# Score products of the later batches: from one fp32 product per step to one stacked fp32r product per head

## The chip, the cores and the metric

The kernel runs on one core of one Trainium2 chip. The metric is the device time of one execution in microseconds (us), as the median of several runs. The core has TensorE (PE; its weight loads are shown apart as PEld), VectorE (DVE), ScalarE (ACT), GpSimd (POOL) and SyncE (SP), whose queue issues nearly all DMAs here.

## The reference

Per batch (4) and head (8) a gated linear attention with a running state over 768 tokens of 40 features, then a mixer over tokens and one over channels. Cut to what is computed:

```python
for t in range(S):
    m_new = max(f[t] + m, i[t]);  f_stab = exp(f[t] + m - m_new);  i_stab = exp(i[t] - m_new)
    C = f_stab * C + i_stab * outer(v[t], k[t]);  n = f_stab * n + i_stab * k[t]
    y[t] = sigmoid(o[t]) * (C @ q[t]) / max(|n . q[t]|, 1)
x = y as [batch, 768, 320]
u = x + (relu(x^T @ w_tok1) @ w_tok2)^T          # 768 -> 256 -> 768
out = u + relu(u @ w_ch1) @ w_ch2                # 320 -> 1536 -> 320
```

## The kernel before

**Attention in steps.** The recurrence is computed in chunks of L = 128 tokens (NC = 6 chunks), and within a chunk in NG = 3 groups of heads (3, 3 and 2 heads). One group of one chunk is a step; a batch has STEPS = 18 of them, numbered m. In batches 1 to 3 (the second to the fourth; the code counts from 0) a step m of batch `ba` goes as follows:

- PE `step_scores`: keys x queries of the group into one PSUM bank. Keys lie in `kd` (heads stacked over partitions, 120 rows); the queries lie in `qz`, zeros outside each head's own rows, so that one fp32 product of 384 (256) columns gives all heads of the step.
- DVE `scores` multiplies the bank by the decay weights in `gb` (which POOL `mask` and ACT `exps` made) and gives p_ready.
- The result is split into three bf16 pieces: ACT `p_high` (first piece), POOL `rest` (subtract it, then cast the second piece), DVE `p_low` (third piece, L860), semaphore p_split.
- PE `step_state` (L1075) adds to the state; DVE `state` fades and adds it.
- PE `step_values` works on step m - 2: the inter-chunk product (L1099) and six bf16 products per head (L1120), after p_split of that step.

Once per chunk come: ACT `chunk_start` (exp of the query decays `gq`, first piece of the values) and `v_middle`, POOL `weigh` (L517), the rest of the values (L551, L556), `scale_q` (queries times decays, L507), `mask` (L499, three) and `x_low` (L521), and DVE `values` (five small instructions).

**Where the steps lie.** Attention of the first batch is a stage of its own (to about 50 us of the span). The mixer of batch b then runs with the attention of batch b + 1 woven in by hand, in the same places on every engine. The channel mixer has 24 slots; in slot s PE does `hidden(s)` (8 fp32r products of 384 columns, L1222 to L1227), then attention step m = s + 2 of the next batch (s - 3 during the first batch's mixer), then `project(s - 1)` (9 fp32r products of 320 columns, L1151). ACT (`h_hi`, L755) and DVE (`h_lo`, L974) split the hidden values in each slot; each engine does its slot's split before its part of the attention step, in strict order. For b > 0, steps 0 and 1 lie in the token mixer before the slots. Steps 0 to 17 and the two values steps after them end in slot 17 (slot 22 of the first batch's mixer); the slots behind have only the mixer. During the first half of the first batch's slots ACT and DVE also split weights (L588, L841).

**Matrix products.** Mixer products are sums of three fp32r products of high and low halves. fp32r halves come from an ACT copy (high) and a subtract (low).

**POOL's order** for a chunk c, written out in `attention` of the POOL block: `weigh(c)`, values' rest, `rest(3c)`, `scale_q(c)`, values' third piece, `rest(3c+1)`, `mask(c+1)`, `rest(3c+2)`, `x_low(c-1)`.

**Loads.** SP issues everything in one order, each load behind the wait for its buffer. `load_chunk(ba, c)` is `load_scores` (keys and three parts of `qz`, 360 KB, buffers of 2 chunks), decays `gb` (3 buffers), `kv` (2), query decays `gq` (3) and queries `qd` (2).

Of the kernel before, what the change touches and what calls it, by code (L numbers as in the profile page):

```python
# [30 lines left out]
GH = 3  # L31
# [20 lines left out]
Q = 3  # L52
SEGMENTS = [(0, 1), (1, 3), (3, NC)]
# [28 lines left out]
def program(nc, qT, kT, kvN, i_gate, f_gate, o_gate, w_tok1, w_tok2, w_ch1, w_ch2, out):  # L82
    ctx = ExitStack()
    with ctx:
# [23 lines left out]

        qd = sb("qd", [ROWS, R, NG, L])
        kd = sb("kd", [ROWS, R, NG, L])  # L110
        qz = sb("qz", [ROWS, R, NG, GH, L])
        kv = sb("kv", [128, R, KV])
        vw = sb("vw", [128, 2, H, E1])

        with ExitStack() as early:
            carry_all = early.enter_context(nc.sbuf_tensor("carry", [NH, S], F32))
        vb = sb("vb", [128, 2, 3, H, E1], BF16)
        gb = sb("gb", [128, Q, H, L])
        gq = sb("gq", [ROWS, Q, NG, L])
        pb = sb("pb", [128, NG, 3, GH, L], BF16)  # L120
# [7 lines left out]
        gp = sb("gp", [3 * NH, S], BF16)  # L128
        g_mid = sb("g_mid", [NH, S], BF16)
        eye = sb("eye", [128, 128], BF16)  # L130
        above = sb("above", [128, L], BF16)
        pick = sb("pick", [3 * NH, NH], BF16)
        pick_q = sb("pick_q", [3 * NH, NG * GH, D], BF16)
# [12 lines left out]
        rows_p = pb[0:NH, :, :, :, :].rearrange("p r a h t -> p (r a h t)").bitcast(F32)  # L146
        f_row, i_row = rows[:, 0:S], rows[:, S:2 * S]
        G_row, A_row = rows_p[:, 0:S], rows_p[:, S:2 * S]
# [15 lines left out]

        def scores_bank(ba, m):

            return [pS, pC[0]][m % 2] if ba == 0 else pS
# [12 lines left out]
        gq_in = [sem(f"gq_in{i}") for i in range(Q)]  # L180
# [109 lines left out]
        def gq_fills(ba, c):  # L290

            return (ba - 1) * (1 if c % Q == 0 else 2) + (1 if c <= Q else 2)
# [11 lines left out]
        def _(sp):  # L304
# [3 lines left out]
            def load_scores(ba, c):  # L308

                n = NC * ba + c  # L310
                r = c % R
                if n >= R:
                    sp.wait_ge(s_mm, NG * (n - R + 1))
                ready = qk_in[r]
                queries = qT[ba, c]
                sp.dma_start(kd[:, r], kT[ba, c]).then_inc(ready, 16)
# [26 lines left out]
            def load_inter(ba, c):  # L343
# [3 lines left out]
                if ba > 0:  # L347
                    last_ba, last_c = (ba, c - Q) if c > Q else (ba - 1, c if c == Q else c + Q)
# [942 lines left out]
```

## Time and profile before

| | us |
|---|---|
| median of 3 runs | 457.97 (457.73 to 460.65) |
| profiled execution: time | 460.83 |
| profiled execution: span | 459.1 |
| TensorE's granted clock, mean | 0.996 of full |

The span is from the first to the last instruction in the trace; the time of that execution is 1.7 us more. The profile gives for each engine the busy time, a chain of work that ended last (followed back from the last instruction to what released each step), groups of instructions by line, and for each group the idle time before it. TensorE is clocked at its full level (2.4 GHz) in every stretch used here.

### The profile page before, as it was taken

The numbers are of one execution on the slowest core, as the hardware profiler recorded it, in microseconds if no ns is written. First come the engines' busy times: TensorE is split into PE (matmuls) and PEld (weight loads), VectorE is DVE, ScalarE is ACT, GpSimd is POOL, SyncE is SP. The second block draws the span as 40 slices with busy tenths as digits, with TensorE's granted clock in tenths as the row PEclk, the third lists the DMA queues.
The fourth block names the chain that finished last, engine by engine and source line by source line (L and its number), as shares of the span: only waits on it lengthen the run. The fifth ranks groups of instructions, "written<-read, shape, count | busy, mean of one in ns | idle before, by whom it ended". The sixth has DMA issues, their size and how long they took to land.

```text
span 459.1 us, 9511 instructions
## 1 busy us (share of the span) xinstructions
PE 440.7 (96%) x3463; PEld 407.9 (89%) x3463; DVE 259.1 (56%) x592; ACT 209.4 (46%) x517; POOL 209.1 (46%) x293
## 2 busy tenths in 40 slices
PE   7899989998999998999999998999999998999996
PEld 3587878998999997999999997899999997999996
DVE  8588965678865346776663236677674326222212
ACT  3665449665555247655552136755552213211120
POOL 7524410888886242988871204698883000000000
PEclk9899999999999999999999999999999999999999
DMA  7666991343344414544344013444410010000101
GB/s 215 191 172 192 348 256 39 104 115 129 95 134 136 140 44 115 148 127 131 127 152 141 1 44 87 144 135 140 126 60 1 1 43 1 0 2 0 45 1 43
DMA packets 36617, 47.38 MB, mean 103 GB/s; under 512 B 3357, under 2 KB 29083, under 8 KB 36571
## 3 DMA queue, kind: packets, MB, share of 16 engines
q1 hardware_dynamic: 35674, 45.76, 33.1%
q10 hardware_dynamic: 896, 1.02, 0.6%
q8 instruction: 28, 0.46, 0.4%
q14 instruction: 19, 0.15, 0.1%
HBM read 42.73 MB, written 4.03 MB: 102 GB/s over the span
## 4 chain that ended last, share of the span: by engine, by line
PE 83%; issue 6%; DVE 4%; ACT 3%; POOL 2%; DMA 1%; ACTq 0%; DVEq 0%; POOLq 0%
PE pC L1151 32%; PE pA L1222 7%; PE pA L1223 7%; PE pA L1224 7%; PE pS L1063 6%; PE pA L1151 5%; PE pY L1120 4%; PE pA L1226 3%; PE pA L1227 3%; PE pY L1099 2%; PE pN L1075 2%; DMA x<-o_gate_dram 1%; PE pA L1181 1%; POOL vw L517 1%; DVE pb L860 1%
## 5 line engine op out<-in xcount | busy, mean ns | idle before, releaser
L974 DVE SCALAR_TENSOR_TENSOR h_lo<-pA,h_hi 128x384 fp32r<-128x384 f32 x96 | 53.5, 557 | 148.0 <-ACT h_hi L755 147.9
L755 ACT ACTIVATE h_hi<-pA 128x384 fp32r<-128x384 f32 x96 | 46.9, 489 | 138.7 <-PE pA L1227 138.6
L1151 PE MATMUL pC<-wc_hi,h_hi 128*128 128x320 f32 x288 | 94.1, 327 | 0.8 <-DVE wc_lo L841 0.8
L1151 PE MATMUL pC<-wc_lo,h_hi 128*128 128x320 f32 x288 | 88.7, 308 | 0.0
L1151 PE MATMUL pC<-wc_hi,h_lo 128*128 128x320 f32 x288 | 88.5, 307 | 0.0
L489 POOL TENSOR_TENSOR gb<-gb,pb 128x384 f32<-128x384 f32 (+1 forms) x54 | 51.7, 957 | 65.7 <-ACT pb L623 65.4
L1222 PE MATMUL pA<-uT_hi,wc_hi 128*128 128x384 f32 x192 | 65.3, 340 | 1.9 <-DVE uT_hi L952 1.9
L1223 PE MATMUL pA<-uT_lo,wc_hi 128*128 128x384 f32 x192 | 64.7, 337 | 0.0
L1224 PE MATMUL pA<-uT_hi,wc_lo 128*128 128x384 f32 x192 | 64.3, 335 | 0.0
L1151 PEld LDWEIGHTS pC<-wc_hi,h_hi 128*128 128x128 f32 x288 | 54.0, 188 | 2.1 <-DVE h_lo L974 1.1
L1151 PEld LDWEIGHTS pC<-wc_lo,h_hi 128*128 128x128 f32 x288 | 54.2, 188 | 0.1
L1151 PEld LDWEIGHTS pC<-wc_hi,h_lo 128*128 128x128 f32 x288 | 54.0, 188 | 0.0
L613 ACT ACTIVATE gb<-gb,aT 128x128 f32<-128x128 f32 x144 | 47.6, 392 | 1.5 <-POOL gb L499 1.5
L1063 PE MATMUL pS<-qz,kd 120*128 120x384 f32 (+1 forms) x126 | 47.1, 454 | 0.0
L623 ACT ACTIVATE pb<-gb 128x384 bf16<-128x384 f32 (+1 forms) x54 | 26.4, 489 | 36.0 <-DVE gb L851 35.5
L860 DVE TENSOR_TENSOR pb<-gb,pb 128x384 bf16<-128x384 f32 (+1 forms) x54 | 38.6, 716 | 0.1
L1222 PEld LDWEIGHTS pA<-uT_hi,wc_hi 128*128 128x128 f32 x192 | 36.0, 187 | 3.0 <-DVE uT_hi L952 2.9
L521 POOL TENSOR_TENSOR x_lo<-x,x_hi 128x320 fp32r<-128x320 f32 x24 | 21.5, 896 | 33.4 <-ACT x_hi L647 33.4
L1224 PEld LDWEIGHTS pA<-uT_hi,wc_lo 128*128 128x128 f32 x192 | 36.0, 188 | 0.0
L1223 PEld LDWEIGHTS pA<-uT_lo,wc_hi 128*128 128x128 f32 x192 | 36.0, 188 | 0.0
L499 POOL TENSOR_SCALAR_AFFINE_SELECT gb<-gb 128x384 f32<-128x384 f32 (+1 forms) x54 | 29.8, 581 | 5.9 <-DMA gb<-g_dram 5.9
L851 DVE TENSOR_TENSOR gb<-pS,gb 128x384 f32<-128x384 f32 (+1 forms) x63 | 31.8, 504 | 1.1 <-PE pS L1063 0.8
(128 smaller groups left out, 885.0 us busy)
## 6 DMA issues: line engine op xcount, KB each, us to landing
gb<-g_dram SPq DMA_DIRECT2D x18, 512.0 KB, 4.0
kv<-kvN_dram SPq DMA_DIRECT2D x24, 324.0 KB, 4.1
kd<-kT_dram SPq DMA_DIRECT2D x24, 180.0 KB
qz<-qT_dram SPq DMA_DIRECT2D x72, 60.0 KB
out_dram<-u SPq DMA_DIRECT2D x24, 160.0 KB, 1.9
qd<-qT_dram SPq DMA_DIRECT2D x20, 180.0 KB, 2.6
gq<-g_dram SPq DMA_DIRECT2D x45, 60.0 KB
wc_raw<-w_ch_dram SPq DMA_DIRECT2D x6, 384.0 KB, 5.8
```

The source lines that it names most:

```text
L489: nc.gpsimd.tensor_tensor(tile, tile, pb[:, g, 0, 0:HEADS[g], :], ALU.subtract).then_inc(p_rest, 1)
L499: nc.gpsimd.affine_select(out=tile, in_=tile, compare_op=ALU.is_ge, fill=NEG, base=0, pattern=[[0, HEADS[g]], [1, L]], channel_multiplier= ...
L613: last = nc.scalar.activation(tile, tile, ACT.Exp, bias=aT[:, c, bass.ds(head, 1)])
L755: nc.scalar.activation(h2[0][:, slot % 2], pA[slot % 2][:, 0:HALF], ACT.Relu).then_inc(h2_hi, 1)
L851: nc.vector.tensor_tensor(tile, scores_bank(ba, m)[:, 0:n * L].rearrange("p (h t) -> p h t", h=n), tile, ALU.mult).then_inc(p_ready, 1)
L860: nc.vector.tensor_tensor(pb[:, g, 2, 0:n, :], gb[:, c % Q, GH * g:GH * g + n, :], pb[:, g, 1, 0:n, :], ALU.subtract).then_inc(p_split, 1)
L974: nc.vector.scalar_tensor_tensor(h2[1][:, slot % 2], pA[slot % 2][:, 0:HALF], 0.0, h2[0][:, slot % 2].bitcast(F32), ALU.max, ALU.subtract) ...
L1063: mm(scores_bank(ba, m)[:, 0:n * L], kd[0:n * D, r, g, :], qz[0:n * D, r, g, 0:n, :].rearrange("p h t -> p (h t)"), start=True, stop=True) ...
L1151: ins = mm(dst, a[p], b[q], start=first and n == 0, stop=last and n == 2)
L1222: mm(dst, wc1[0][:, t, f], uh[:, t, cols], start=t == 0, stop=False)
L1223: mm(dst, wc1[0][:, t, f], ul[:, t, cols], start=False, stop=False)
L1224: mm(dst, wc1[1][:, t, f], uh[:, t, cols], start=False, stop=False)
```

## The change

Batch 0 stays as it was (`first_scores`). For batches 1 to 3:

- **Data.** A new input `kq` holds, per batch, chunk and group, keys and queries head by head, 120 rows each. By features the stack is 0:40, 0:24, 0:40, 24:40, for keys and queries alike. Once rows 0 to 39 of the keys and rows 64 to 103 of the queries are replaced by their low halves, one product over the 120 rows sums low x high, high x low and (rows 40 to 63 and 104 to 119) high x high of a head.
- **Per step.** SP loads 120 x 768 floats (360 KB) into `kq_raw` (one buffer per group, so three). ACT `step_high` copies them to `kq_stack` as fp32r. POOL `low_keys` subtracts in rows 0 to 39, DVE `step_low` in rows 64 to 103. PE `step_scores` waits for both and then makes one fp32r product of 128 columns per head.
- **Where.** Step k is prepared two steps ahead (`prepares`): at m = 2 step 3, at m = 3 steps 4 and 5, then step m + 2; at m = 16 to 18 steps 0 to 2 of the next batch. The first three steps of batch 1 are prepared by POOL alone (`prepare_first`).
- **Loads.** `load_chunk` is now decays, two steps, values, third step, query decays, queries. `gq` has two buffers instead of three from batch 1 on; the first batch has `gq_first` as its third. Of batch 1 only chunk 0 is loaded ahead of `load_o(1)`, not two chunks.
- **Memory.** `qz`, `kd` and tensors that only the first batch uses lie under the new ones.

```diff
+FIRST_PREPARED = 3
+PREPARES_AT = 2
+TWO_AT = 3
+K_LOW, Q_LOW = slice(0, D), slice(64, 64 + D)
...
+        kq_raw = sb("kq_raw", [ROWS, NG, 2, GH, L])
+        kq_stack = sb("kq_stack", [ROWS, NG, 2, GH, L], F32R)
...
+        def prepares(ba, m):
+
+            if m < PREPARES_AT:
+                return []
+            steps = [m + 1] if m < TWO_AT else [m + 1, m + 2] if m == TWO_AT else [m + 2]
+            n = STEPS + (FIRST_PREPARED if ba < B - 1 else 0)
+            return [later(ba, k) for k in steps if k < n and later(ba, k) >= FIRST_PREPARED]
...
+            def load_step(ba, m):
+
+                c, g = divmod(m, NG)
+                k = later(ba, m)
+                if k < NG:
+                    sp.wait_ge(s_mm, STEPS)
+                elif k < NG + FIRST_PREPARED:
+                    sp.wait_ge(kq_first, 2 * (k - NG + 1))
+                else:
+                    sp.wait_ge(kq_lo, k - NG - FIRST_PREPARED + 1)
+                    sp.wait_ge(kq_low_keys, k - NG - FIRST_PREPARED + 1)
+                sp.dma_start(kq_raw[:, g], kq[ba - 1, c, :, g]).then_inc(kq_in[g], 16)
...
+            def load_two_steps(ba, c):
+                load_decays(ba, c)
+                load_step(ba, NG * c)
+                load_step(ba, NG * c + 1)
+
             def load_rest(ba, c):
-                if ba > 0:
-                    load_decays(ba, c)
                 load_values(ba, c)
+                load_step(ba, NG * c + 2)
                 if c > 0:
-                    load_inter(ba, c)
+                    load_query_decays(ba, c)
+                    load_queries(ba, c)
...
             def rest(ba, m):
 
+                sixteen_bits(ba, m)
+                for k in prepares(ba, m):
+                    low_keys(k)
...
+            def low_keys(k):
+
+                raw, stack = step_tiles(kq_raw, k % NG), step_tiles(kq_stack, k % NG)
+                pool.wait_ge(kq_hi, k - FIRST_PREPARED + 1)
+                nc.gpsimd.tensor_tensor(stack[0][K_LOW], raw[0][K_LOW], stack[0][K_LOW].bitcast(F32),
+                                        ALU.subtract).then_inc(kq_low_keys, 1)
...
+                for k in prepares(ba, m):
+                    step_high(k)
                 c = chunk_at(ba, m, 1)
                 if c is not None:
                     x_high(ba, c)
+
+            def step_high(k):
+
+                g = k % NG
+                act.wait_ge(kq_in[g], 16 * (k // NG + 1))
+                act.wait_ge(s_mm, STEPS + k - NG + 1)
+                nc.scalar.activation(kq_stack[:, g, :, 0:HEADS[g], :], kq_raw[:, g, :, 0:HEADS[g], :],
+                                     ACT.Copy).then_inc(kq_hi, 1)
...
+                if ba > 0:
+                    for k in prepares(ba, m):
+                        step_low(k)
+
+            def step_low(k):
+
+                raw, stack = step_tiles(kq_raw, k % NG), step_tiles(kq_stack, k % NG)
+                dve.wait_ge(kq_hi, k - FIRST_PREPARED + 1)
+                nc.vector.tensor_tensor(stack[1][Q_LOW], raw[1][Q_LOW], stack[1][Q_LOW].bitcast(F32),
+                                        ALU.subtract).then_inc(kq_lo, 1)
...
+                if k < FIRST_PREPARED:
+                    pe.wait_ge(kq_first, 2 * (k + 1))
+                else:
+                    pe.wait_ge(kq_lo, k - FIRST_PREPARED + 1)
+                    pe.wait_ge(kq_low_keys, k - FIRST_PREPARED + 1)
+                pe.wait_ge(p_ready, STEPS + k)
+                for j in range(HEADS[g]):
+                    last = mm(scores_bank(ba, m)[:, j * L:(j + 1) * L], kq_stack[:, g, 0, j, :], kq_stack[:, g, 1, j, :],
+                              start=True, stop=True)
+                last.then_inc(s_mm, 1)
```

## Rows read from the trace of the kernel before

**Rows 1.** The page, part 1: busy us (share of the span) xinstructions.
```profile
PE 440.7 (96%) x3463; PEld 407.9 (89%) x3463; DVE 259.1 (56%) x592; ACT 209.4 (46%) x517; POOL 209.1 (46%) x293
```

**Rows 2.** The page, part 4: share of the chain that ended last, by engine.
```profile
PE 83%; issue 6%; DVE 4%; ACT 3%; POOL 2%; DMA 1%; ACTq 0%; DVEq 0%; POOLq 0%
```

**Rows 3.** Stretches: length, busy us of each engine, clock, DMA share, GB/s.
```profile
52.50:77.00 24.50, 21.99 (x141) 20.46 (x141) 16.34 (x35) 14.96 (x30) 4.58 (x7) 1.00 0.75 210
...
97.50:110.00 12.50, 12.14 (x108) 11.30 (x103) 10.26 (x18) 7.31 (x19) 10.96 (x14) 1.00 0.47 129
...
207.30:219.80 12.50, 12.50 (x118) 11.84 (x118) 8.43 (x20) 7.13 (x20) 10.48 (x14) 1.00 0.40 130
...
245.00:267.80 22.80, 22.80 (x170) 22.68 (x167) 6.13 (x14) 5.35 (x13) 3.70 (x6) 1.00 0.19 57
```

**Rows 4.** TensorE's timeline: start us, length us, line, operation, tile, shapes, count.
```profile
169.13 0.38 PE L1181 MATMUL pA<-ident,u 128*128 128x128 f32 x2
...
169.35 0.27 PE L1183 MATMUL pA<-ident,u 128*128 128x128 f32 x1
...
190.01 0.59 PE L1063 MATMUL pS<-qz,kd 80*128 80x256 f32 x2
...
190.44 0.37 PE L1075 MATMUL pN<-vw,kv 128*120 128x123 f32 x2
...
199.02 0.81 PE L1063 MATMUL pS<-qz,kd 120*128 120x384 f32 x2
...
199.67 0.37 PE L1075 MATMUL pN<-vw,kv 128*120 128x123 f32 x2
```

**Rows 5.** Waits of GpSimd from 293.18 to 349.32 us (fourth batch).
```profile
POOL gb L489 <- ACT pb L623: 7.0, 9, 2.1
POOL x_lo L521 <- ACT x_hi L647: 2.7, 4, 0.7
```

**Rows 6.** The same from 92.38 to 149.95 us (second batch), x_lo's line alike.
```profile
POOL gb L489 <- ACT pb L623: 9.0, 9, 2.1
...
```

**Rows 7.** Timeline of GpSimd, in brackets idle time before and its releaser.
```profile
92.38 0.92 POOL L489 TENSOR_TENSOR gb<-gb,pb 128x384 f32<-128x384 f32 x1 [1.78 <-ACT pb L623]
...
149.95 0.67 POOL L489 TENSOR_TENSOR gb<-gb,pb 128x256 f32<-128x256 f32 x1 [2.10 <-ACT pb L623]
...
197.86 1.25 POOL L489 TENSOR_TENSOR gb<-gb,pb 128x384 f32<-128x384 f32 x1
...
199.63 1.00 POOL L507 TENSOR_TENSOR qd<-qd,gq 120x384 f32<-120x384 f32 x1
...
200.59 0.82 POOL L556 TENSOR_TENSOR vb<-kv,vb 128x328 bf16<-128x328 f32 x1
...
293.18 0.92 POOL L489 TENSOR_TENSOR gb<-gb,pb 128x384 f32<-128x384 f32 x1 [0.30 <-ACT pb L623]
...
349.32 0.68 POOL L489 TENSOR_TENSOR gb<-gb,pb 128x256 f32<-128x256 f32 x1 [2.10 <-ACT pb L623]
```

**Rows 8.** Groups of GpSimd by form: busy, mean ns | idle before.
```profile
L468 POOL TENSOR_TENSOR u<-u 32x384 f32<-32x384 f32 x1 | 1.0, 986 | 0.1
...
L468 POOL TENSOR_TENSOR u<-u 32x256 f32<-32x256 f32 x1 | 0.7, 717 | 0.1
```

**Rows 9.** TensorE's value products of step 16, second and fourth batch.
```profile
151.92 0.61 PE L1120 MATMUL pY<-vb,pb 128*128 128x41 bf16 x18
...
351.29 0.61 PE L1120 MATMUL pY<-vb,pb 128*128 128x41 bf16 x18
```

**Rows 10.** ScalarE's weight split by form; line L860, min/median/max ns.
```profile
L588 ACT ACTIVATE wc_hi<-wc_raw 128x768 fp32r<-128x768 f32 x6 | 4.9, 835 | 0.0
...
L860 DVE TENSOR_TENSOR pb<-gb,pb x54: 408/552/1284, 83.4 to 352.3; 128x384 bf16<-128x384 f32 x36, 128x256 bf16<-128x256 f32 x18
```

More of the change, by code:

```diff
@@ L79, in step_in, with program @@
     return slot - BEHIND if b == 0 else slot + AHEAD
-def program(nc, qT, kT, kvN, i_gate, f_gate, o_gate, w_tok1, w_tok2, w_ch1, w_ch2, out):
+def program(nc, qT, kT, kq, kvN, i_gate, f_gate, o_gate, w_tok1, w_tok2, w_ch1, w_ch2, out):
     ctx = ExitStack()
@@ L163, in program, with gq_at, step_tiles @@
         pN = bank("pN")
+        def gq_at(ba, c):
+            if ba == 0:
+                return gq_first[:, :, :] if c % Q == R else gq[:, c % Q]
+            return gq[:, c % R]
+        def step_tiles(tensor, g):
+            return [tensor[:, g, side, 0:HEADS[g], :] for side in range(2)]
         def scores_bank(ba, m):
@@ L179, in program @@
         gb_in = [sem(f"gb_in{i}") for i in range(Q)]
-        gq_in = [sem(f"gq_in{i}") for i in range(Q)]
+        gq_in = [sem(f"gq_in{i}") for i in range(R)]
+        kq_in = [sem(f"kq_in{i}") for i in range(NG)]
+        kq_hi = sem("kq_hi")
+        kq_lo = sem("kq_lo")
+        kq_low_keys = sem("kq_low_keys")
+        kq_first_hi = sem("kq_first_hi")
+        kq_first = sem("kq_first")
         g_out = sem("g_out")
@@ L401, in _ @@
             sp.wait_ge(g_pad_out, 16)
-            for c in range(R):
-                load_chunk(1, c)
+            load_chunk(1, 0)
             def store(b, half):
@@ L413, in _ @@
                     load_o(b + 1)
-                    for c in range(R, NC):
+                    for c in range(1 if b == 0 else R, NC):
                         load_chunk(b + 1, c)
                 if b < B - 2:
-                    load_scores(b + 2, 0)
+                    load_two_steps(b + 2, 0)
                 store(b, 0)
@@ L548, in attention @@
                         pool.wait_ge(v_weighed, (NC - 1) * ba + c + 1)
+                    if n == NC:
+                        for m in range(FIRST_PREPARED):
+                            prepare_first(m)
                     pool.wait_ge(v_hi, n - NC + 1)
@@ L562, in attention @@
                         x_low(ba, c - 1)
+                for k in prepares(ba, STEPS):
+                    low_keys(k)
                 x_low(ba, NC - 1)
@@ L1125, in attention @@
             def attention(ba, m):
-                if m < STEPS:
+                if m < STEPS and ba > 0:
                     step_scores(ba, m)
                 if ba == 0:
+                    if m < STEPS:
+                        first_scores(m)
                     if m in (1, 4):
@@ L1265, in rows, with stacked @@
         return np.ascontiguousarray(padded.reshape(B, NG, ROWS, NC, L).transpose(0, 3, 2, 1, 4))
+    def stacked(a):
+        order = np.r_[0:D, 0:64 - D, 0:D, 64 - D:D]
+        heads = np.concatenate([a[1:], np.zeros((B - 1, NG * GH - H, S, D), np.float32)], axis=1)
+        return heads.reshape(B - 1, NG, GH, NC, L, D).transpose(0, 3, 5, 1, 2, 4)[:, :, order]
     def by_partition(w, k):
@@ L1275 @@
     arrays = {
-        "qT": rows(q), "kT": rows(k),
+        "qT": rows(q), "kT": rows(k), "kq": np.ascontiguousarray(np.stack([stacked(k), stacked(q)], axis=4)),
         "kvN": np.ascontiguousarray(np.concatenate([tokens(k).reshape(B, S, DM), values.reshape(B, S, H * E1)], axis=2)),
```

129 lines of the change are left out of this document (79 added, 50 removed).

## The prediction

> **What bounds the kernel now.** I read the profile in four steps. First the busy shares and the chain that ended last [rows 1, 2]: TensorE is busy for 96% of the span and holds 83% of the chain, so on average it is the bound. An average doesn't say what a change in one stage is worth, so second the table of stretches [rows 3]. The second, third and fourth batch's attention steps run inside the channel slots of the batch before them, three slots (one chunk of attention) in some 12.5 us. In such a stretch TensorE is busy all the time, VectorE 8.4 to 10.3 us, ScalarE about 7 us, and GpSimd 10.5 to 11.0 us. In the slots after the last attention step (245 to 267.8 us) TensorE is still full and all others are nearly idle. So the reader should see two things: TensorE sets the pace by a small margin, and GpSimd comes right behind it, with some 2 us free in 12.5. Third, the waits of GpSimd from the first to the last of its `rest` steps that matter [rows 5, 6], and its timeline [rows 7]: they say how much of its free time could be used. Fourth, TensorE's starts [rows 4], for the price of one score step.
>
> **TensorE's part of the change.** Before, a score step of three heads is one fp32 product of 384 columns that runs as two records; from its start at 199.02 to the next instruction's at 199.67 it takes 0.65 us, and one of two heads takes 190.44 - 190.01 = 0.43 us [rows 4]. After, it is one fp32r product of 128 columns per head, each with its own weight load of 128 columns. No row shows fp32r with 128 columns. The nearest below are the transposes, 128x128 f32, one record each: three starts in 0.22 us, so 0.11 us each [rows 4]. The bound above is the fp32 rate, 0.65/3 = 0.22 us per head, which is no saving at all. I take 0.11, because there too each product has a weight load of 128 columns of four bytes. That gives 0.33 and 0.22 us per step; over 54 steps (36 of three heads, 18 of two) TensorE is freed of 36 x 0.32 + 18 x 0.21 = 15.3 us. If TensorE stayed the bound, this would be the gain. A chunk of attention would then take 12.5 - 0.32 - 0.32 - 0.21 = 11.65 us.
>
> **What the others get.** Every step of the 54 now has to be split. ScalarE copies 120x768 (two heads: 120x512) to fp32r; the weight split of 128x768 takes 0.84 us [rows 10]. Three per chunk add about 2.3 us to its 7: 9.4 of 11.65, hidden. VectorE subtracts 40 partitions x 384 (256) from SBUF to SBUF. The nearest row is the subtract of the third piece, L860: 0.41 at best, median 0.55, 1.28 us at worst [rows 10]. Three add 1.5 us at the median, 3.3 at the worst, to 8.4 (10.3 in the second batch's stretch, where weights are split too) [rows 3]. Just hidden, and in the second batch close to its own bound. GpSimd subtracts 40x384 twice and 40x256 once per chunk. That few partitions are used should not help: its subtract of 32x384 takes 0.99 us and of 32x256 0.72 [rows 8], as long as the 120x384 product, 1.00 us, which takes 0.96 from its start at 199.63 to the next at 200.59 [rows 7]. So I take 0.96 and, scaled, 0.68 us: 2.6 us per chunk.
>
> **GpSimd becomes the bound.** In the fourth batch, from `rest(3)` at 293.18 to `rest(17)` at 349.32 [rows 7], 56.14 us pass, of which GpSimd waited 9.7 [rows 5]; 0.3 of that lies before the first instruction, so 46.7 us are work. The third batch has the same pattern. In the second batch, 92.38 to 149.95 is 57.57 us, with 9.0 + 2.7 = 11.7 us of waits [rows 5, 6] of which 1.8 lie before the first; 47.7 us of work. In these stretches 15 subtracts are added (keys of steps 4 to 18, five of them of two heads): 10 x 0.96 + 5 x 0.68 = 13.0 us. 46.7 + 13.0 = 59.7 is more than 56.1, and far more than the 52.1 us that TensorE would want (56.1 less the saving of 14 steps, 14 x 15.3/54 = 4.0). So GpSimd is late, and the waits it had are used up.
>
> What is late next: `rest(16)` gives the second piece of step 16, VectorE subtracts (`p_low`), and TensorE's value products of step 16 wait for it; after these come one more slot and step 17, which no cover shortens. Before, these products start at 351.29 and 151.92 [rows 9]. After, fourth batch: `rest(3)` starts about 0.6 late, since ScalarE has 0.84 us more to do before it and gets back about 0.2 from the shorter score steps: 293.8. Of the last batch only steps up to 17 are prepared, so 14 subtracts lie before `rest(17)`, and `rest(16)` is done at 293.8 + 46.7 + 12.0 = 352.5. `p_low` 0.9 us (between 0.55 and 1.28): 353.4, which is 2.1 us later than 351.29. Third batch: the same work up to `rest(16)`, so 2.1 us too. Second batch: 93.0 + 47.7 + 12.0 + 0.9 = 153.6, against 151.92, so 1.7 us. Sum 5.9 us.
>
> **Contention on top.** GpSimd's subtract of 128x384 takes 0.92 us at 293.18 and 1.25 at 197.86 [rows 7], and VectorE's subtract 0.55 or up to 1.28 [rows 10]: the two engines stretch each other when both read from SBUF. VectorE's 15 new subtracts per batch run beside a GpSimd that is never idle. Below, 0 us (they fall on instructions that were not stretched); above, 0.33 us each, 5 us per batch. Most GpSimd forms of the trace keep their time, so I take a quarter, 1.3 us per batch, 3.9 in all.
> The Trainium skill, page "SBUF — State Buffer", section "Who interferes with whom", says that a VectorE instruction with two SBUF inputs excludes a GpSimd instruction that reads SBUF for its whole length. The rows show less, 0.33 us of a 0.55 us instruction; by the page the delay would be the whole length of each, which is the fourth rival below.
>
> **What costs nothing.** DMA: per chunk 3 loads of 360 KB replace 360 KB, 0.7 MB more in 12 us, so 130 [rows 3] becomes about 190 GB/s; while the weights are loaded, 210 GB/s take 0.75 of the DMA engines' time [rows 3], so some 280 are to be had. Deadlines: the load of step k waits for the split of step k - 3, about three slots (12 us) before the split of k; what stands between them on the SyncE queue (decays, values, query decays, which now wait for the chunk two back instead of three) waits for work at least one slot earlier than the need. If that cover went, each late load would cost what it is late, in every chunk. The three prepared steps of the second batch (a copy and two subtracts each, some 8.5 us on GpSimd) lie between its masks and the first slot with attention, where it is nearly idle (busy 4.6 of the 24.5 us from 52.5 to 77 us [rows 3]); they are hidden. The new memory layout and the split of the SyncE loads move no work of the first batch.
>
> **Rivals.**
> (1) *GpSimd is no bound, TensorE stays it* (the other side). For it: the profile's spans on GpSimd are rough, and only 40 of 128 partitions are used. If a subtract cost 0.3 us, the stretch would be 46.7 + 15 x 0.3 = 51.2 us, no more than TensorE wants. Then all 15.3 us are saved: 443. Between, it decides at about 0.82 us per subtract: there GpSimd's delay of 2 us per batch is gone, and below it each 0.1 us gives 1.4 us per batch. Against: the rows of 32 partitions.
> (2) *GpSimd is the bound, but it comes out even.* The subtracts cost 0.8 us, or `rest` gets shorter where VectorE is shifted away from it, or ScalarE is not late: 458, within 453 to 462.
> (3) *fp32r with 128 columns runs no faster than fp32.* TensorE keeps its 12.5 us per chunk; GpSimd needs 10.5 + 2.6 = 13.1 anyway, so the end is the same but for a start later by 0.2 us per batch. It lies inside the forecast, and so this price, which could be all of the gain, hardly matters.
> (4) *Full exclusion.* Each of VectorE's new subtracts stops GpSimd for its whole length, 0.50 us on average (0.55 and 0.41): 15 x 0.50 = 7.5 us per batch, 458.0 + 5.9 + 22.5 = 486. In the same direction: in the second batch VectorE becomes a bound itself.
>
> **The numbers.** The profiled execution has a span of 459.1 us and a time of 460.8; the median of the runs is 458.0. The sum of changes is 5.9 + 3.9 = 9.8 us: span 468.9, and for the median 458.0 + 9.8 = 467.8, rounded 468. Chances: forecast 0.60 (460 to 479, with (3) in it), rival (1) with the cases between it and even 0.15, (2) 0.17, (4) 0.08. A measurement of this kernel tells about 1% from no change (453.4 to 462.6). Faster: 0.15 and a bit of (2), 0.16. Same: most of (2) and the low edge of the forecast, 0.22. Slower: 0.62. The range must leave out no more than 2 in 10: it drops most of (1) and (4), so 454 to 480.
>
> **What would show it.** In the changed kernel's trace: in the stretches of three slots GpSimd busy 12.5 us and more of 13 to 14, its waits in the stretch of 56 us gone from 9.4 us to under 2, and TensorE with gaps of 1 to 2 us per chunk, put down to VectorE (`p_low`, `h_lo`) or ScalarE. Starts of the three fp32r products 0.11 us apart. The slots after the attention as long as before. GpSimd's new subtracts at 0.96 us from start to start. It is wrong if they take under 0.8 us, or if GpSimd still waits some microseconds per chunk; then the time falls by what TensorE saved.

## The result and the profile after

| | before | after |
|---|---|---|
| median, us (four runs each) | 459.31 (457.73 to 461.18) | 515.64 (513.56 to 517.94) |
| ratio, 95% interval | | 1.1231 [1.1193, 1.1268] |
| span of the profiled execution | 459.1 | 513.7 |
| TensorE's mean granted clock | 0.996 | 0.959 |

The ratios below leave out two slow executions, one of e14 (690.0 us at a granted clock of 0.554) and one of e12 (481.4 us).

The change costs 12%. The forecast was 468 with a range of 454 to 480: the direction was right, the size was not. First the page of the changed kernel, part 1 (busy time, to be read beside [rows 1]) and part 4 (the chain that ended last, beside [rows 2]).

```profile
PE 450.0 (88%) x3499; PEld 422.3 (82%) x3499; DVE 309.9 (60%) x643; ACT 241.1 (47%) x568; POOL 277.9 (54%) x353
...
PE 52%; DVE 18%; ACT 11%; issue 10%; POOL 6%; DMA 1%; ACTq 0%; DVEq 0%; POOLq 0%
```

TensorE no longer sets the pace by itself: it holds 52% of the chain, 83% before. Its idle time is span less busy time: 459.1 - 440.7 = 18.4 us before, 513.7 - 450.0 = 63.7 us after. That is 45.3 of the 54.6 us of added span. The other 9.3 are busy time, although the score products got shorter. The granted clock is large enough to account for it: (1 - 0.959) x 513.7 = 21.1 us of full-speed time were lost, part of them while TensorE stood, against 1.8 before.

The stretches of the changed kernel (columns as in [rows 3]): a chunk of the third batch's attention, one of the fourth's, the fourth batch from `rest(3)` to `rest(17)`, and the 24.5 us in which the first three steps are prepared.

```profile
244.00:259.90 15.90, 12.46 (x119) 11.79 (x119) 11.30 (x24) 8.63 (x22) 13.88 (x18) 1.00 0.55 147
...
345.00:360.90 15.90, 12.42 (x112) 11.84 (x111) 11.34 (x23) 8.50 (x22) 13.89 (x18) 0.89 0.54 147
...
330.03:403.76 73.73, 61.76 (x555) 60.33 (x555) 53.28 (x108) 38.40 (x94) 61.68 (x75) 0.92 0.46 124
...
62.50:87.00 24.50, 22.46 (x154) 20.78 (x155) 17.11 (x32) 18.39 (x37) 16.78 (x19) 1.00 0.56 162
```

One chunk takes 15.9 us, and no engine fills it: TensorE 12.4, VectorE 11.3, ScalarE 8.6, GpSimd 13.9. In the kernel before a steady chunk takes 12.6 us, and TensorE is busy for all of it:

```profile
305.48:318.07 12.59, 12.59 (x118) 11.93 (x118) 9.13 (x20) 6.79 (x18) 10.52 (x16) 1.00 0.40 120
```

The slots behind the attention kept their length. So the loss is made in the steps: 3.3 us x 4 chunks x 3 batches = 40 us, and most of the rest in the first steps of each batch.

Then the waits: TensorE's over the whole span, and GpSimd's from `rest(3)` to `rest(17)` of the fourth batch (beside [rows 5]).

```profile
PE pY L1238 <- DVE den L1019: 14.3, 6, 2.6
...
PE pY L1238 <- DVE x L1014: 6.9, 6, 2.4
...
POOL gb L564 <- ACT pb L726: 5.0, 7, 1.6
POOL kq_stack L595 <- ACT kq_stack L752: 4.1, 4, 1.0
```

Before, the first two lines together were 1.9 us; now they are 21.2. TensorE now stands at its inter-chunk product until VectorE has read the bank of values. GpSimd itself still waits for 9.1 us, where the forecast wanted under 2.

The chain of waits inside one chunk of the third batch says what sets 15.9 us (start, us, what; pieces of the sequencers, of "issue" and some short ones are left out).

```profile
223.47 0.62 ACT kq_stack L752
...
224.12 0.41 DVE kq_stack L1047
...
224.82 0.56 DVE h_lo L1098
225.38 0.46 DVE gb L964
...
226.50 2.02 DVE pb L973
228.52 0.40 DVE x L1014
...
230.26 0.76 DVE kq_stack L1047
...
231.05 0.56 DVE h_lo L1098
231.61 0.34 DVE gb L964
...
232.30 0.97 ACT gb L716 x3
...
234.05 0.74 ACT kq_stack L752
...
234.86 0.34 POOL kq_stack L595
...
236.20 0.87 POOL x_lo L617
237.06 0.71 POOL vw L613
...
237.84 1.12 POOL kv L650
...
239.37 0.62 ACT kq_stack L752
```

It is a ring that comes back to the same ScalarE copy after 239.37 - 223.47 = 15.90 us, over ScalarE, VectorE, ScalarE, GpSimd and back, **without one TensorE instruction**. Before, the chain of the steady chunk (305.48 to 318.07 us) was TensorE's throughout. The preparation holds five places in the ring. The chain shows only part of some of them: GpSimd's subtract of 234.86 has 0.34 us there, but runs for 1.38 (timeline below). From the start of each to the start of the ring's next work they hold 0.65 + 0.70 + 0.79 + 0.81 + 1.34 = 4.3 us. And one old instruction in the ring, the third piece (`p_low`, L973), takes 2.02 us, where [rows 10] has 0.55 as its median. Of the 54 third pieces nine took 2.02 to 2.42 us, four of them in the third batch and four in the fourth, one per chunk.

The timeline around it shows what happened to that instruction.

```profile
226.32 0.91 POOL L655 TENSOR_TENSOR vb<-kv,vb 128x328 bf16<-128x328 f32 x1
226.50 2.02 DVE L973 TENSOR_TENSOR pb<-gb,pb 128x384 bf16<-128x384 f32 x1
...
227.20 0.90 POOL L564 TENSOR_TENSOR gb<-gb,pb 128x384 f32<-128x384 f32 x1
...
228.17 0.72 POOL L566 CAST pb<-gb 128x384 bf16<-128x384 f32 x1
228.44 0.48 DVE L1014 TENSOR_TENSOR x<-pY,x 128x320 f32<-128x320 f32 x1
...
229.29 0.76 PE L1238 MATMUL pY<-st,qd 120*128 120x123 f32 x2 [2.64 <-DVE den L1019]
...
234.86 1.38 POOL L595 TENSOR_TENSOR kq_stack<-kq_raw,kq_stack 40x384 fp32r<-40x384 f32 x1 [1.03 <-ACT kq_stack L752]
```

VectorE's instruction began 0.18 us after GpSimd's of 226.32 and ended at 228.52, about 0.4 us after the end of GpSimd's next one (227.20 to 228.10): it was held through two GpSimd subtracts that followed each other without a gap. Behind it stood the value instructions, and behind them TensorE, 2.64 us.

TensorE's own part came as forecast: three score products at 216.77, the next instruction at 217.06, 0.29 us where 0.33 was forecast and [rows 4] has 0.65.

```profile
216.77 0.45 PE L1202 MATMUL pS<-kq_stack 120*128 120x128 f32 x3
217.06 0.32 PE L1214 MATMUL pN<-vw,kv 128*80 128x82 f32 x2
```

### The profile page after: what moved, and what is told of

Same layout as the page of the kernel before. It is cut to its first block, busy times and chain, and to the rows that moved or that the text cites. A ratio compares the mean times of both kernels' runs of the same rounds, so it can differ in the third digit from the quotient of the medians.

```text
span 513.7 us, 9866 instructions
## 1 busy us (share of the span) xinstructions
PE 450.0 (88%) x3499; PEld 422.3 (82%) x3499; DVE 309.9 (60%) x643; ACT 241.1 (47%) x568; POOL 277.9 (54%) x353
## 4 chain that ended last, share of the span: by engine, by line
PE 52%; DVE 18%; ACT 11%; issue 10%; POOL 6%; DMA 1%; ACTq 0%; DVEq 0%; POOLq 0%
PE pC L1292 21%; PE pA L1363 4%; PE pA L1364 4%; DVE pb L973 4%; PE pA L1365 4%; PE pA L1292 4%; ACT kq_stack L752 3%; DVE kq_stack L1047 3%; DVE gb L964 3%; ACT gb L716 2%; PE pA L1368 2%; PE pA L1367 2%; DVE h_lo L1098 2%; PE pY L1259 2%; POOL vw L613 2%
## 5 line engine op out<-in xcount | busy, mean ns | idle before, releaser
L1292 PE MATMUL pC<-wc_hi,h_hi 128*128 128x320 f32 x288 | 97.3, 338 | 7.6 <-DVE u L1111 6.8
L1292 PE MATMUL pC<-wc_hi,h_lo 128*128 128x320 f32 x288 | 92.2, 320 | 0.0
L1292 PE MATMUL pC<-wc_lo,h_hi 128*128 128x320 f32 x288 | 92.0, 320 | 0.0
L564 POOL TENSOR_TENSOR gb<-gb,pb 128x384 f32<-128x384 f32 (+1 forms) x54 | 47.5, 879 | 56.5 <-ACT pb L726 56.5
L1047 DVE TENSOR_TENSOR kq_stack<-kq_raw,kq_stack 40x384 fp32r<-40x384 f32 (+1 forms) x51 | 39.3, 775 | 53.2 <-ACT kq_stack L752 52.8
L1363 PE MATMUL pA<-uT_hi,wc_hi 128*128 128x384 f32 x192 | 68.6, 357 | 2.4 <-DVE uT_hi L1076 2.3
L595 POOL TENSOR_TENSOR kq_stack<-kq_raw,kq_stack 40x384 fp32r<-40x384 f32 (+1 forms) x51 | 56.2, 1105 | 13.0 <-ACT kq_stack L752 13.0
L973 DVE TENSOR_TENSOR pb<-gb,pb 128x384 bf16<-128x384 f32 (+1 forms) x54 | 49.3, 913 | 0.1
L1238 PE MATMUL pY<-st,qd 120*128 120x123 f32 (+1 forms) x102 | 20.9, 286 | 21.1 <-DVE den L1019 14.3
L752 ACT ACTIVATE kq_stack<-kq_raw 120x768 fp32r<-120x768 f32 (+1 forms) x51 | 38.4, 758 | 0.0
```

The lines of the kernel that those rows point to most:

```text
L564: nc.gpsimd.tensor_tensor(tile, tile, pb[:, g, 0, 0:HEADS[g], :], ALU.subtract).then_inc(p_rest, 1)
L595: nc.gpsimd.tensor_tensor(stack[0][K_LOW], raw[0][K_LOW], stack[0][K_LOW].bitcast(F32), ALU.subtract).then_inc(kq_low_keys, 1)
L752: nc.scalar.activation(kq_stack[:, g, :, 0:HEADS[g], :], kq_raw[:, g, :, 0:HEADS[g], :], ACT.Copy).then_inc(kq_hi, 1)
L973: nc.vector.tensor_tensor(pb[:, g, 2, 0:n, :], gb[:, c % Q, GH * g:GH * g + n, :], pb[:, g, 1, 0:n, :], ALU.subtract).then_inc(p_split, 1)
L1047: nc.vector.tensor_tensor(stack[1][Q_LOW], raw[1][Q_LOW], stack[1][Q_LOW].bitcast(F32), ALU.subtract).then_inc(kq_lo, 1)
L1292: ins = mm(dst, a[p], b[q], start=first and n == 0, stop=last and n == 2)
```

## The experiments

One figure is used throughout: the length of one chunk in steady state (three slots of the third or fourth batch). Times are medians; "against" is the kernel before, run beside it. That one moved between 458.7 and 460.9 us from experiment to experiment, so small differences between experiments are taken from the ratios.

**1. One instruction of the preparation at a time (e1, e2, e3), and all three (e4).** Each cut instruction stays where it is, with its waits, but works on 2 columns of one head; the low halves or copies of the rest are left out. e4 does it on all three engines.

```diff
- nc.gpsimd.tensor_tensor(stack[0][K_LOW], raw[0][K_LOW], stack[0][K_LOW].bitcast(F32),
+ nc.gpsimd.tensor_tensor(stack[0][K_LOW, 0:1, 0:2], raw[0][K_LOW, 0:1, 0:2], stack[0][K_LOW, 0:1, 0:2].bitcast(F32),
```

> Left out: GpSimd's subtraction of the keys' low halves, but for two columns per step; its waits and semaphores stay, so the low keys are missing from the scores. Theory S (saturation: GpSimd's own work of 14.1 us per chunk sets the pace, as the prediction said): nearly all of the 56 us comes back, 455 to 462 us. Theory W (a ring of in-order waits through ScalarE, GpSimd and VectorE, in which every one of the new instructions stands, 15.9 us per chunk): only its own length on the ring and what it stretches come back, about 2 to 2.5 us per chunk of 16, so 515 goes to 475 to 483.

> Left out: VectorE's subtraction of the queries' low halves, but for two columns per step; waits and semaphores stay. Theory S: VectorE has room, little changes but for less stretching of GpSimd, 505 to 515 us. Theory W: its 0.67 and 0.76 us stand on the ring in each chunk and the subtract of the third piece, now 2.0 us, gets shorter: 1.4 to 2 us per chunk, 485 to 495.

> Left out: ScalarE's copy of the stack to fp32r, but for two columns per tile; the low halves are computed from what is in the buffer. Theory S: nothing, 510 to 516 us. Theory W: two copies of 0.74 and 0.62 us stand on the ring in each chunk, 1.4 us per chunk of 16, so 490 to 496.

> Left out: the copy and both subtractions, but for two columns each; all waits, the loads of 360 KB per step and the products per head stay. Shows what TensorE alone would gain. Both theories: 441 to 446 us, 459 less the 15.3 us of the prediction, if no load is late. If loads were late or SyncE's queue in the way, it would stay above 450.

Measured, against 459.14: e1 504.2, 1.0969 [1.0861, 1.1078]; e2 500.9, 1.0897 [1.0836, 1.0957]; e3 505.8, 1.1005 [1.0933, 1.1077]; e4 478.7, 1.0415 [1.0322, 1.0508]. GpSimd's subtract, by the forecast the whole loss, gives back 11 us of 56. Each engine's part gives 10 to 15, all three 37. If the amount of GpSimd's work set the pace, taking this part of it away would have freed the kernel; it did not, so it was not the bound. A steady chunk takes 14.75 us in e1, 15.0 in e2 and 15.3 in e3, so each part returns 1.2, 1.0 and 0.6 us of the 1.34, 1.49 and 1.46 that it held in the ring. That supports the ring and shows its limit: theory W had named 475 to 483, 485 to 495 and 490 to 496, and the runs came out 21, 6 and 10 us above. Presumably another path of nearly the same length takes over when this one gets shorter; which one was not looked for. And 20 us stay when nothing but stubs of the preparation are left (e4; both theories had 441 to 446).

**2. Where the preparation stands (e5, e6, e11).** e5 prepares step m + 2 from the start on instead of catching up at m = 3; e6 also makes both low halves one step later (m + 1) than the copy; e11 is e4 with e5's places. e5 and e6 leave nothing out.

```diff
-PREPARES_AT = 2
+PREPARES_AT = 1
-            steps = [m + 1] if m < TWO_AT else [m + 1, m + 2] if m == TWO_AT else [m + 2]
+            steps = [m + 2]
```

> The changed kernel with each step prepared two steps ahead throughout (step 3 at m = 1 instead of m = 2, step 4 at m = 2, step 5 at m = 3). Theory R (the place of the preparation: in slots 0 and 1 step 3's copy stands on ScalarE behind a table load and the sigmoid, and TensorE waits 3.8 and 4.2 us for it; at m = 3 two steps are prepared at once): 8 to 13 us come back, 503 to 508 us. If the time is set by the later chunks alone, as a backlog that builds up anyway: within 3 us of 515.6.

> The changed kernel with each step's copy two steps ahead throughout, and both subtractions one step after the copy (step k's low halves at m = k - 1), so that VectorE and GpSimd no longer stop at once for ScalarE's copy, with h_lo and x_low queued behind. Same work, same result. Theory R (the waits for the copy, 53 us on VectorE and 13 us on GpSimd, carry the loss): 485 to 500 us. If the loss is in the work and in the shared reads of VectorE and GpSimd (theory P), which this leaves as they are: 505 to 516.

> Copy and both subtractions cut to two columns (left out as in the run with 478.7 us), and each step prepared two steps ahead throughout. What is late there besides the work: at step 3 TensorE waits some 3 us, at step 4 some 2.5 us in each later batch. Theory R: 3 x 4 us come back, 463 to 469 us. If it only moves the wait on: 474 to 479.

e5 514.0, 1.1199 [1.1167, 1.1232]; e6 550.9, 1.1946 [1.1842, 1.205]; e11 476.1, 1.0323 [1.0213, 1.0433]. An earlier place gives back 2 us of 56, so the place is not the cause; the later one of e6 is much worse. In e6 SyncE's queue shows why (SyncE's timeline; the second figure is the time that the issues took with the waits between them):

```profile
231.73 8.37 SPq L376 DMA_DIRECT2D kq_raw<-kq_dram  x2
240.18 0.35 SPq L398 DMA_DIRECT2D kv<-kvN_dram  x1
...
246.01 1.09 SPq L412 DMA_DIRECT2D gq<-g_dram  x3
```

The load of a step waits until both low halves of the step three back are made; `kv` and the query decays `gq` stand behind it in the same queue. ScalarE then waited for `gq` 12 times, 26.9 us in all. In the changed kernel no such wait appears, so this is a cost that lies close by, not the one that was paid.

**3. The clock (e8).** Six bf16 products of 512 columns, whose result nobody reads, ahead of the scores of steps 5, 8, ..., 17, where TensorE stands.

> The changed kernel with six bf16 products of 512 columns (0.22 us each, 1.3 us) ahead of the score products of steps 5, 8, 11, 14 and 17, whose result is overwritten: 15 places, 20 us of TensorE time, most of it where TensorE would stand still a little later. Theory C (after each such pause the granted clock falls to 1.2 GHz for some microseconds; a mean of 0.959 over 513.7 us means 42 us at half clock, 21 us of lost work, half of it on the path): the clock rises above 0.98 and the time falls by 3 to 12 us. Without C: the time rises by up to 10 us.

515.3, 1.1175 [1.1066, 1.1284]. The clock of the profiled execution rose from 0.959 to 0.972, the time stayed, though two runs can't exclude a few us. The first two lines of stretches above say the same: at clock 1.00 and at 0.89 a chunk takes 15.90 us. TensorE stands because the ring is late, then its granted clock falls, and in these chunks that costs nothing, since the ring is longer than TensorE's own work.

**4. Two inputs against one (e7, e9, e10).** e7 is e4 with VectorE's stub as a copy. e9 and e10 add 51 instructions of 40x384 to VectorE in the kernel *before*, at the places of the new subtracts, with results nobody reads: a subtract of two SBUF inputs, and a maximum of one input and a constant.

```diff
+ nc.vector.tensor_tensor(gp[0:D].bitcast(F32)..., thrice, thrice, ALU.subtract)       # e9
+ nc.vector.tensor_scalar_max(gp[0:D].bitcast(F32)..., thrice, 1.0)                     # e10
```

> As the run in which copy and both subtractions were cut to two columns (478.7 us), but VectorE's instruction is a copy with one SBUF input instead of a subtract with two. Left out: the same as there. Theory P (VectorE's instructions with two SBUF inputs are held until a pause between GpSimd's instructions; there 40x2 takes 438 ns on average and up to 1.34 us): the 51 instructions fall to some 0.16 us, 14 us less on VectorE, of which about half is on the path: 469 to 474 us. Without P: 478.

> The kernel before, with one more VectorE instruction behind each of the steps 2 to 18 of the later batches (51 in all): a subtract of 40x384 whose two inputs and output lie in SBUF; nobody reads what it writes, nothing waits for it, it waits for nothing. By the prediction's price (0.55 us each, hidden): 458 to 461. Theory P: held by GpSimd and holding it, 1 us and more on average, and behind it h_lo and the scores are late: 464 to 480.

> The same as the run with one more subtract per step, but the added instruction is a maximum with a constant, 40x384, with one SBUF input. Theory P: 458 to 462, clearly less than with two inputs. Without P (only VectorE's time counts): the same as with two inputs.

e7 479.0, 1.0437 [1.0305, 1.0568]; e9 467.7, 1.0191 [1.0138, 1.0245]; e10 462.7, 1.0084 [1.0033, 1.0136]. The line of the added instruction in e9 and then in e10 (min/median/max ns):

```profile
L930 DVE TENSOR_TENSOR gp<-ident x51: 541/748/1270, 86.3 to 360.3; 40x384 f32<-40x384 f32 x51
```

```profile
L930 DVE TENSOR_SCALAR gp<-ident x51: 533/536/540, 86.0 to 354.3; 40x384 f32<-40x384 f32 x51
```

With one input it is never held; with two it is held up to 0.73 us. The subtract of two inputs costs 467.7 - 462.7 = 5.0 us more than the maximum of one, and merely having one more instruction on VectorE 4.0 us, in a kernel where VectorE is busy for 56%. With two and three runs each of these is uncertain by 2 to 4 us, and the two instructions differ in their operation as well. The copy of e7 has one input too, and was held: 159 to 1351 ns. So it isn't the count of inputs alone. (The Trainium skill, page "SBUF — State Buffer", section "Who interferes with whom", names copies beside instructions of two inputs among those that can contend with GpSimd; e7 agrees. It says that operations with a scalar can as well, when their operands meet certain conditions, and e10's maximum was not held.) The stub of e4, 40x2, says that a small size is no protection: 0.15 us at best, 1.34 at worst.

**5. VectorE's state sum behind its values (e12).** e11 with `st` moved behind `values`.

> As the run with small work and early preparation, and VectorE's state sum (two SBUF inputs, 0.35 us, up to 2.08 us when GpSimd runs without a pause) moved behind the reading of the values bank. Left out: the same. Theory P, with the loop from a chunk's middle score step through VectorE to TensorE's next values: in two of three chunks this instruction holds TensorE up 1.7 us and lets its clock fall: another 8 to 15 us less than the run before it, 450 to 458. Without P: no change against it.

Two executions, 474.3 and 481.4 us, too few for a ratio. Neither comes near the 450 to 458 that theory P had named; beside e11's 476.1 no gain is seen.

**6. The low halves out altogether (e14, e15, e19).** e14 has no low half on VectorE; ScalarE's copy and GpSimd's subtract are whole. e15 has none on either engine and a cut copy. e19 is e15 with the copy whole. Products, loads and their order stay; whoever waited for the low halves waits for the copy. No row of e14 is shown; only its times are used.

> Leaves out VectorE's low halves of the queries altogether (no instruction, where e2 kept one of 2 columns); ScalarE's copy and GpSimd's subtract are whole. Theory H (held instructions): the 51 cut instructions of e11, 0.16 us alone, cost VectorE 16.5 us beyond that because each one was held while GpSimd worked, up to 1.34 us, and they pushed the score and value instructions into GpSimd's later work. Then it is the number of VectorE's instructions in the loop that costs, not their size, and without them the time falls well below e2's 500.9: about 485. Theory L (loads: SyncE's queue and two instead of three buffers of the query decays): nothing but the tiny instruction itself is saved, 500 within 3.

> Leaves out both low halves altogether and cuts ScalarE's copy to 2 columns; the stacked products, their loads and the order of the loads stay. Theory H: what kept e4 and e11 at 476 to 479 were the two cut instructions per step on VectorE and GpSimd; without them the time is that of TensorE's bound with the shorter products, 443 to 452. Theory L: the loads and their order are untouched, so the time stays at 470 to 478. In between, both take part.

> e15 with ScalarE's copy whole: no low halves on VectorE and GpSimd. It divides the 36 us between e15 (460) and e14 (496) into ScalarE's part and that of GpSimd's subtract. Theory V: a copy of 0.84 us lies once per step in ScalarE's chain of the slot and delays the decay tiles and the high halves of the hidden layer, 5 to 15 us: 465 to 475, the rest of the 36 is GpSimd's subtract and the waits between the two.

e14 496.0 (three runs), 1.0768 [1.0727, 1.0809]; e15 459.9, 0.9987 [0.9959, 1.0016], both against 460.4; e19 468.6, 1.0227 [1.0175, 1.0278] against 459.0. So the loss can be added up from the bottom, by the ratios, each step uncertain by 2 to 3 us: e15 0, ScalarE's copy +11 (e19), GpSimd's subtract +25 (e14), VectorE's subtract +21 (the whole kernel). From the top the same parts gave 10, 11 and 15 (e3, e1, e2). The difference between two stubs and nothing (e15 to e4, 19 to 20 us) is what instructions of almost no work cost in an order of waits.

And e15, in which TensorE has every bit of its saving and the others almost none of the price, is no faster than before. Where did 15 us go? The chain of one chunk of e15:

```profile
306.38 0.53 DVE gb L965
306.92 0.20 DVE stn L995
...
307.38 0.70 issue
308.07 1.27 DVE pb L974
309.34 0.41 DVE x L1015
...
310.12 0.46 PE pY L1240 x2
```

At one place per chunk the chain leaves TensorE: from the score products VectorE goes to the scores, the state sum, the third piece (1.27 us, held) and the values, and TensorE's inter-chunk product waits 0.51 us for these. In the steady chunks of the kernel before there is no such wait. The same place there, first VectorE's third piece with GpSimd's subtract beside it, then VectorE's last reading of the bank of values and TensorE's inter-chunk product:

```profile
320.42 0.55 DVE L860 TENSOR_TENSOR pb<-gb,pb 128x384 bf16<-128x384 f32 x1
320.45 1.30 POOL L489 TENSOR_TENSOR gb<-gb,pb 128x384 f32<-128x384 f32 x1 [0.25 <-ACT pb L623]
...
321.48 0.17 DVE L906 SCALAR_TENSOR_TENSOR den<-pY,den 128x8 f32<-128x8 f32 x1
...
322.86 0.39 PE L1099 MATMUL pY<-st,qd 120*128 120x123 f32 x2
```

VectorE was done 322.86 - 321.65 = 1.2 us before TensorE came. In e15 the two subtracts start in the other order:

```profile
307.96 0.97 POOL L564 TENSOR_TENSOR gb<-gb,pb 128x384 f32<-128x384 f32 x1
308.07 1.27 DVE L974 TENSOR_TENSOR pb<-gb,pb 128x384 bf16<-128x384 f32 x1
```

Before, VectorE started 0.03 us ahead, and GpSimd took 1.30 us instead of 0.92 [rows 7]; in e15 GpSimd starts 0.11 us ahead, and VectorE takes 1.27 instead of 0.55. The state sum, 0.35 us before, takes 0.90 in e15, and it too starts just after a GpSimd instruction (0.06 us). Together VectorE is 1.27 us later. That uses up the 1.2 us, and the shorter products, which bring TensorE to this place sooner, do the rest of the wait. The order decides throughout. Of the third pieces just ahead of the values, one per chunk, 20 in the two kernels began within 0.12 us of GpSimd's subtract: six times VectorE was ahead, by about 0.04 us, and took 0.55 us; 14 times GpSimd was ahead, by 0.05 to 0.12 us, and VectorE took 1.26 to 1.28. Ten of these 14 are in e15. So a shift of a tenth of a microsecond in the start decides whether VectorE or GpSimd is held. That it was the shorter products that shifted it in e15 is likely, but was not tested by itself.

**7. The hold taken away (e16, e17, e18).** GpSimd's own subtract in `rest`, which both kernels have and beside which the third piece is held, cut to 2 columns: in e15 (e16), in the kernel before (e17) and in the changed kernel (e18).

```diff
- nc.gpsimd.tensor_tensor(tile, tile, pb[:, g, 0, 0:HEADS[g], :], ALU.subtract).then_inc(p_rest, 1)
+ small = tile[0:1, 0:1, 0:2]
+ nc.gpsimd.tensor_tensor(small, small, pb[0:1, g, 0, 0:1, 0:2], ALU.subtract).then_inc(p_rest, 1)
```

> e15 (no low halves of the stack, ScalarE's copy cut) and on top GpSimd's own subtract of `rest`, which both kernels have (128x384, 0.93 us), cut to 2 columns. In e15 TensorE stood for 0.5 to 0.8 us in every chunk before the state product, waiting for VectorE's value instruction, and VectorE came late because its state sum took 0.90 (0.35 at best) and its third piece 1.27 us (0.55) while GpSimd ran subtracts and products. Theory V (what is left of the missing gain is the loop TensorE - VectorE, stretched by GpSimd): 443 to 450. Theory L (loads and their order): e15's 460 stays. Theory G (GpSimd's occupied time): GpSimd works only 10.5 of 12.4 us here, so nothing changes, 460.

> The kernel before with the same subtract of `rest` cut to 2 columns. Its TensorE waited only 1.9 us for VectorE's values in the whole span, so theory V expects almost nothing here: 455 to 458. If the cut alone gave 10 us or more here too, e16 would say nothing about the change.

> The changed kernel, its preparation whole, with GpSimd's subtract of `rest` cut to 2 columns: GpSimd is freed of 2.5 us per chunk, about as much as its low halves of the keys cost it (e1: 11 us saved). If the loss came from GpSimd's occupied time, this is e1 again: 502 to 506. If it comes from VectorE being held at the third piece, which stands between the score and the value products and runs beside exactly this subtract, it saves more: 480 to 490.

e16 450.9, 0.9833 [0.9805, 0.9862]; e17 457.0, 0.9955 [0.993, 0.9979]; e18 502.9, 1.0966 [1.0882, 1.1049], all against 459.0. The cut takes 9.0 us from e15 as the medians stand, 7 by the ratios, and 2.0 from before, where TensorE's three waits for the values (1.9 us) are gone: with shorter products VectorE's loop decides, with the old ones it hardly does. One chunk in steady state of e16, e15, e19 and e4 (length, busy us of PE, PEld, DVE, ACT, POOL, clock, DMA share, GB/s), to be read beside the 12.59 us of before:

```profile
311.60:323.30 11.70, 11.70 (x124) 11.68 (x123) 7.65 (x21) 7.12 (x22) 9.16 (x15) 1.00 0.77 206
```

```profile
304.40:316.80 12.40, 11.89 (x121) 11.72 (x120) 9.54 (x21) 7.07 (x21) 10.31 (x15) 1.00 0.77 200
```

```profile
312.00:325.10 13.10, 11.66 (x119) 11.49 (x116) 9.56 (x20) 8.69 (x22) 10.37 (x15) 1.00 0.72 177
```

```profile
317.67:331.17 13.50, 11.84 (x121) 11.68 (x120) 11.48 (x24) 6.95 (x21) 10.67 (x18) 1.00 0.69 175
```

In the four with the stacked products TensorE works 11.7 to 11.9 us, the forecast's 11.65; only in e16 does it work all the time. From e15 on the length is set by the others: 12.4, 13.1, 13.5, 15.9, with no engine full in any. e18's miss is worth as much as e16's hit: in the whole kernel the same cut gives 12.7 us, about what e1's does, and that is the number of the theory of GpSimd's occupied time (502 to 506), not of the hold (480 to 490). The third piece was held less (1.16 us at most, 2.42 in the whole kernel), and the steady chunk fell only from 15.9 to 15.1 us. So in the whole kernel the hold is one part of the ring among several. The run can't tell a shorter hold from a shorter list of GpSimd, because the cut makes both.

e16 is still 8 us above the 443 that TensorE alone would want, though its steady chunk is at 11.7. The rest should lie in the first steps of each batch. ScalarE waited 1.1 us for `gq` in the fourth batch, and TensorE once waited 1.8 us for a copy of the preparation (waits of e16, 270 to 302 us):

```profile
PE pS L1205 <- ACT kq_stack L754: 1.8, 1, 1.8
...
ACT gq L698 <- DMA gq<-g_dram: 1.1, 1, 1.1
```

That these account for the 8 us was not shown.

## Why the prediction was wrong, point by point

**TensorE's part: right.** 0.33 us per step of three was forecast and 0.29 measured, a chunk of 11.65 forecast and 11.7 measured (e16).

**"GpSimd becomes the bound": wrong, and this is the step that carried the forecast.** Its sum of work was good: 46.7 + 13.0 gave about 60 us from `rest(3)` to `rest(17)`, and 61.7 were measured (the new subtracts took 1.10 us on average, 0.96 and 0.68 were forecast). But the stretch took 73.7 us, not 60, with 9.1 us of waits. The forecast compared amounts of work, engine by engine, and took the largest. What bounds the kernel is a ring of waits through ScalarE, VectorE and GpSimd, each of which works its list in order, and a ring's length is no engine's busy time. e1 shows it: without GpSimd's part 45 of 56 us stay. The forecast had named this sign of its own error, a GpSimd that still waits some microseconds per chunk, but had tied it to the gain of 15 us; the sign came with the loss.

**"ScalarE: hidden", "VectorE: just hidden": wrong by the same error.** ScalarE had 5.8 us free in each chunk of 12.6, and its copy costs 9 to 11 us by itself (e19); VectorE's subtract 15 to 21 (e2, e14). Each was priced by whether it fits into the engine's free time. It should have been priced by what stands behind it: behind the copy, the high half of `h` and the decay tiles; behind VectorE's subtract, `h_lo` and the next scores. A row of the kernel before gave a first hint (TensorE's timeline, fourth batch):

```profile
297.64 0.46 PE L1099 MATMUL pY<-st,qd 120*128 120x123 f32 x2 [0.36 <-DVE x L901]
```

This wait came once in the third and once in the fourth batch (0.36 us each) and once in the second (1.22 us), always early; the steady chunks have none. There the measure is the distance that the lines at 321.48 and 322.86 show: VectorE's loop had 1.2 us to spare, and 0.4 us in the chunks in which its third piece was held (in the fourth batch the one at 307.94, 1.27 us). The shorter products take part of that, and the new subtract, which stands ahead of `h_lo` and the scores, 0.70 us (in the ring above), before any further hold is counted. These 0.4 to 1.2 us, and not VectorE's 3.5 us of free time, were the room that the change had.

**Contention: the mechanism right, its size and its side wrong.** The forecast took 0.33 us x a quarter, 3.9 us in all, and put it on GpSimd. Where it costs time, it is VectorE that is held. [rows 10] had shown 0.55 and 1.28 us for the third piece, a hold of 0.73; in the changed kernel it is up to 1.87 (median 0.67, largest 2.42 us), and the new subtract took up to 2.87 us. e9 measured 5.0 us for the subtract of two inputs over the maximum of one with GpSimd's load as before, and e16 7 to 9 us for the hold of an instruction that was always there.
The cut of e16 also takes 0.9 us from each of GpSimd's `rest` steps, so the 7 to 9 are the hold and that together; the longest third piece fell from 1.28 (e15) to 0.71 us.
Which side pays depends on who starts first, as the 20 pairs of experiment 6 show.
The Trainium skill, page "SBUF — State Buffer", section "Who interferes with whom", says that the order of issue decides which of the two engines blocks. The traces agree. The 2.02 us above go further: they are a wait for two GpSimd instructions in a row. The forecast had read only one side of it, GpSimd kept out by VectorE (the fourth rival, 486).

**DMA and deadlines: right in steady state, not at the start.** 206 GB/s and a full TensorE in e16 say that loads and their new order cost nothing there. In the first steps of a batch they may cost some of e16's 8 us, and e6 shows how near the queue was.

**The clock: not in the sum, and rightly so.** It fell (0.959), but e8 and the two chunks at 1.00 and 0.89 show that the time did not follow it.

**Rival (1), TensorE stays the bound, 443:** its condition, cheap subtracts, was the wrong condition. Even with no subtracts at all the time is 460 (e15). **Rival (4)** was nearest in size and still 30 us short. **The first three steps**, prepared by GpSimd alone, were hidden as forecast: GpSimd is busy 16.8 of the 24.5 us there, and the first third piece starts at 82.9 us, against 83.4 in [rows 10].

**Not settled:** how the 56 us divide, since the parts depend on the order in which they are taken away, how much of them is hold and how much is the mere length of the new instructions, and which path takes over when one of them is shortened (e18, e12). No version tried beats both kernels with its work whole.

## What to carry to other kernels

Before an engine's saving is booked, look for the longest loop that does not run through it, and measure how much that loop has to spare: in a steady stretch, the time between the last instruction that the bounding engine will need and the moment at which it needs it. Here it was 0.4 to 1.2 us per chunk. Work that is added to that loop, and what the saving itself takes from the distance, is paid in full beyond it, however idle the engines are. Price an added instruction by who stands behind it in that engine's order, and try it first as a stub: if the stub alone costs time, no faster version of it will help.

## What the hardware did unexpectedly

- VectorE subtracts of two SBUF inputs were held through several GpSimd instructions in a row: the third piece 2.02 us here and 2.42 at most, against 0.55, the new subtract 2.87 at most. Cutting the latter to 2 columns did not free it: 0.15 us at best, 1.34 at worst (e4).
- With VectorE's subtract 0.03 us ahead of GpSimd's, GpSimd's took 1.30 us and VectorE's 0.55; with GpSimd's 0.11 us ahead, 0.97 and 1.27.
- A maximum of one input stayed at 0.53 to 0.54 us in 51 of 51 (e10); a copy of one input did not (0.16 to 1.35, e7).
- GpSimd's subtract of 40x384 took 0.99 us at the median, as much as its product of 120x384 in [rows 7].
- fp32r products of 128 columns started about 0.1 us apart, 0.29 us for three.
